# Mean square spread by a constant matrix, inverse root on VectorE, in a three-stage fp32 kernel

## The reference, cut to what matters

```
qn, kn = q / norm over rows, k / norm over rows
a = softmax(kn.T @ qn / tau)                 # 256 x 256
x = v @ a                                    # 6016 x 256
x = x / sqrt(mean(x*x over the 256) + 1e-6) * rms_g
g = x @ w1_gate;  y = (g * sigmoid(g) * (x @ w1_val)) @ w1_out
out = (sigmoid(y @ w2_gate) * (y @ w2_val)) @ w2_out
```

## Time and profile before

| what | value |
|---|---|
| device time, median of 3 runs | 1309.73 us (1309.46 to 1310.09) |
| span of the profiled execution | 1307.8 us |
| PE busy | 1295.0 us, 99% |
| DVE busy | 655.3 us, 50% |
| ACT busy | 455.3 us, 35% |
| POOL busy | 37.7 us, 3% |

### The profile page before, as it was taken

One profiled execution on the slowest core, in us unless ns is written; L12 is line 12 of the kernel. 1 busy time (PEld: TensorE's weight loads), 2 busy tenths in 40 slices (PEclk: granted clock), 3 DMA queues, 4 the chain that ended last, 5 costly groups with the idle time before them and its releaser, 6 DMA issues.

```text
span 1307.8 us, 15519 instructions
## 1 busy us (share of the span) xinstructions
PE 1295.0 (99%) x5706; PEld 1067.3 (82%) x5706; DVE 655.3 (50%) x1014; ACT 455.3 (35%) x737; POOL 37.7 (3%) x32
## 2 busy tenths in 40 slices
PE   8999999999999999999999999999999999999998
PEld 7878888888888888888888888888888888889888
DVE  6776544544554554554454455455455455445333
ACT  5453533333332333333333333333333333333322
POOL 0000500000000000000000000000000000000000
PEclk9999999999999999999999999999999999999999
DMA  9910000100100100010010010010010001000000
GB/s 345 315 57 1 1 1 1 33 0 0 32 0 0 32 0 0 8 24 0 0 32 0 0 32 0 0 32 0 0 25 7 0 0 28 1 1 17 1 17 13
DMA packets 60569, 34.43 MB, mean 26 GB/s; under 512 B 50816, under 2 KB 54144, under 8 KB 60544
## 3 DMA queue, kind: packets, MB, share of 16 engines
q1 hardware_dynamic: 60544, 34.09, 8.9%
HBM read 27.92 MB, written 6.16 MB: 26 GB/s over the span
## 4 chain that ended last, share of the span: by engine, by line
PE 98%; DVE 1%; DMA 0%; SPq 0%; POOL 0%; issue 0%; ACT 0%; DVEq 0%
PE ps L661 21%; PE ps L662 21%; PE ps L663 21%; PE ps L779 10%; PE ps L780 10%; PE ps L781 10%; PE ps L727 3%; PE ps L687 1%; DMA qk<-in_k 0%; PE ps L696 0%; PE ps L703 0%; SPq L250 0%; POOL small L296 0%; PE ps L713 0%; DVE w_lo_v L442 0%
## 5 line engine op out<-in xcount | busy, mean ns | idle before, releaser
L596 DVE TENSOR_TENSOR h<-ps,h 128x512 f32<-128x512 f32 (+1 forms) x288 | 196.1, 681 | 328.0 <-PE ps L663 322.2
L390 ACT ACTIVATE h_hi<-h 128x512 fp32r<-128x512 f32 (+1 forms) x288 | 179.6, 624 | 406.9 <-DVE h L596 405.3
L384 ACT ACTIVATE h<-ps 128x512 f32<-128x512 f32 (+1 forms) x288 | 169.9, 590 | 402.5 <-PE ps L663 402.5
L601 DVE TENSOR_TENSOR h_lo<-h,h_hi 128x512 fp32r<-128x512 f32 (+1 forms) x288 | 195.4, 679 | 131.0 <-ACT h_hi L390 127.1
L779 PE MATMUL ps<-h_hi,w_hi_o 128*128 128x512 f32 (+1 forms) x576 | 225.9, 392 | 0.0
L780 PE MATMUL ps<-h_lo,w_hi_o 128*128 128x512 f32 (+1 forms) x576 | 225.8, 392 | 0.0
L781 PE MATMUL ps<-h_hi,w_lo_o 128*128 128x512 f32 (+1 forms) x576 | 225.3, 391 | 0.0
L592 DVE TENSOR_TENSOR h<-ps,h 128x512 f32<-128x512 f32 (+1 forms) x144 | 98.0, 681 | 165.5 <-ACT h L384 164.8
L781 PEld LDWEIGHTS ps<-h_hi,w_lo_o 128*128 128x128 f32 x576 | 110.8, 192 | 23.0
L779 PEld LDWEIGHTS ps<-h_hi,w_hi_o 128*128 128x128 f32 x576 | 110.2, 191 | 23.6
L780 PEld LDWEIGHTS ps<-h_lo,w_hi_o 128*128 128x128 f32 x576 | 110.1, 191 | 21.9
(11 more groups left out here) (111 smaller groups left out, 1321.6 us busy)
## 6 DMA issues: line engine op xcount, KB each, us to landing
v_in<-in_v SPq DMA_DIRECT2D x44, 128.0 KB, 3.2
out<-out_sb SPq DMA_DIRECT2D x44, 128.0 KB, 2.6
qk<-in_q SPq DMA_DIRECT2D x10, 512.0 KB, 7.6
qk<-in_k SPq DMA_DIRECT2D x10, 512.0 KB, 9.1
w_raw_g<-in_moe_w_gate SPq DMA_DIRECT2D x6, 512.0 KB, 7.9
w_raw_v<-in_moe_w_val SPq DMA_DIRECT2D x6, 512.0 KB, 8.0
w_raw_o<-in_moe_w_out SPq DMA_DIRECT2D x6, 512.0 KB, 9.0
qk<-in_q SPq DMA_DIRECT2D x3, 256.0 KB, 2.9
```

Of the source, the lines that this page charges most:

```text
L384: nc.scalar.activation(h[:, slot, 0:w], ps[:, GATE[slot], 0:w], ACT.Sigmoid).then_inc(sig_done, 1)
L390: nc.scalar.activation(h_hi[:, part, 0:w], h[:, slot, 0:w], ACT.Copy).then_inc(hi_done, 1)
L596: nc.vector.tensor_tensor(h[:, slot, 0:w], ps[:, VALUE[slot], 0:w], h[:, slot, 0:w], ALU.mult).then_inc(h_done, 1)
L601: nc.vector.tensor_tensor(h_lo[:, part, 0:w], h[:, slot, 0:w], h_hi[:, part, 0:w].bitcast(F32), ALU.subtract).then_inc(lo_done, 1)
```

## The change

From block 2 on, `add_squares` is followed by a split of the summed squares (`squares_high` on ACT, `squares_low` on DVE). Two matmuls of w columns with a 128x128 matrix of 1/256 as weights (`spread_mean`) put the mean square of each token on all partitions. ACT copies it to SBUF with 1e-6 added (`mean_copy`). DVE makes a first guess of the inverse root from the bits (`root_seed`, on integers), and betters it in three rounds of three instructions (`root_better`). `x_norm` then reads it from SBUF. `sum_squares`, `mean_square`, the power on POOL, `diagonal` and `spread_rms` are left for blocks 0 and 1 alone. The steps in which the pieces stand are moved too, for block 1 as well: `vt_high` and `vt_low` from 1 to 0, `make_x` from 2 to 1, `x_square`, `x_gain` and `add_squares` from 3 to 2, `sum_squares` from 4 to 3, `mean_square`, `diagonal` and `spread_rms` from 5, 6, 7 to 4, 5, 6, `x_norm` from 8 to 9, both `xs_low` to 10. `spread_mean` stands in step 4, `mean_copy` and `root_seed` in 5, the three rounds in 6, 7 and 8. Two tiles are added in SBUF, `mean_r` and `root`.

```diff
@@ -59,6 +61,10 @@
+    def narrow(b):
+        return isinstance(b, int) and b < 2
     def width(b):
@@ -117,12 +123,14 @@
+        mean_r = sb("mean_r", [P, P], F32R)
...
+        root = sb("root", [P, 2, BLOCK])
@@ -302,9 +312,6 @@
                                         ALU.subtract).then_inc(w_lo2_done, 1)
-            with pool.Fori(0, FULL - 2) as b:
-                inverse_rms(b + 2)
-            inverse_rms(FULL)
@@ -336,6 +343,18 @@
                 nc.scalar.activation(sq[:, c, 0:w], ps[:, X[c], 0:w], ACT.Square).then_inc(x_squared, 1)
+            def squares_high(b, dst):
+                w = width(b)
+                act.wait_ge(squares_added, b)
+                nc.scalar.activation(dst[0][:, 0, 0:w], sq[:, 0, 0:w], ACT.Copy).then_inc(sq_hi_done, 1)
+            def mean_copy(b):
+                w = width(b)
+                act.wait_ge(ms_spread, b - 1)
+                nc.scalar.activation(sq[:, 0, 0:w], ps[:, X[0], 0:w], ACT.Copy, bias=1e-6).then_inc(ms_copied, 1)
@@ -392,8 +411,11 @@
             def next_x(mid, end, b, vt):
-                mid[1] = [(vt_high, b, c, vt) for c in range(CC)]
-                mid[3] = [(x_square, b, c) for c in range(CC)]
+                mid[0] = [(vt_high, b, c, vt) for c in range(CC)]
+                mid[2] = [(x_square, b, c) for c in range(CC)]
+                if not narrow(b):
+                    mid[3] = [(squares_high, b, vt)]
+                    mid[5] = [(mean_copy, b)]
@@ -511,12 +533,44 @@
+            def squares_low(b, dst):
+                w = width(b)
+                dve.wait_ge(sq_hi_done, b - 1)
+                nc.vector.tensor_tensor(dst[1][:, 0, 0:w], sq[:, 0, 0:w], dst[0][:, 0, 0:w].bitcast(F32), ALU.subtract)\
+                  .then_inc(sq_lo_done, 1)
+            def root_seed(b):
+                w = width(b)
+                dve.wait_ge(ms_copied, b - 1)
+                nc.vector.tensor_scalar(root[:, 0, 0:w].bitcast(I32), sq[:, 0, 0:w].bitcast(I32), -0.5, float(0x5f3759df),
+                                        ALU.mult, ALU.add).then_inc(root_step, 1)
+            def root_better(b, n):
+                w = width(b)
+                steps = (b - 2) * (1 + 3 * ROOT_ROUNDS) + 1 + 3 * n
+                y, t = root[:, 0, 0:w], root[:, 1, 0:w]
+                dve.wait_ge(root_step, steps)
+                nc.vector.scalar_tensor_tensor(out=t, in0=y, scalar=-0.5, in1=y, op0=ALU.mult, op1=ALU.mult)\
+                  .then_inc(root_step, 1)
+                dve.wait_ge(root_step, steps + 1)
+                nc.vector.tensor_tensor(t, t, sq[:, 0, 0:w], ALU.mult).then_inc(root_step, 1)
+                dve.wait_ge(root_step, steps + 2)
+                nc.vector.scalar_tensor_tensor(out=y, in0=t, scalar=1.5, in1=y, op0=ALU.add, op1=ALU.mult)\
+                  .then_inc(root_step, 1)
             def x_norm(b, c):
                 w = width(b)
-                dve.wait_ge(rinv_spread, b + 1)
+                if narrow(b):
+                    dve.wait_ge(rinv_spread, b + 1)
+                    by = ps[:, X[1], 0:w]
+                else:
+                    dve.wait_ge(root_step, (b - 1) * (1 + 3 * ROOT_ROUNDS))
+                    by = root[:, 0, 0:w]
                 dve.wait_ge(xg_done, b * 2 + c + 1)
-                nc.vector.tensor_tensor(x_raw[:, c, 0:w], x_raw[:, c, 0:w], ps[:, X[1], 0:w], ALU.mult)\
-                  .then_inc(xn_done, 1)
+                nc.vector.tensor_tensor(x_raw[:, c, 0:w], x_raw[:, c, 0:w], by, ALU.mult).then_inc(xn_done, 1)
@@ -572,6 +626,7 @@
             nc.vector.tensor_copy(ones_r[:, :], ones[:, :]).then_inc(ones_r_done, 1)
+            nc.vector.tensor_scalar(mean_r[:, :], ones[:, :], 1.0 / C, None, ALU.mult).then_inc(mean_r_done, 1)
             dve.wait_ge(g_loaded, 16)
@@ -604,14 +659,16 @@
             def next_x(extras, b, vt):
-                for j, work in {0: [(turn_v, b, 0), (turn_v, b, 1)],
-                                1: [(vt_low, b, 0, vt), (vt_low, b, 1, vt)],
-                                3: [(x_gain, b, 0), (x_gain, b, 1), (add_squares, b)],
-                                5: [(mean_square, b)],
-                                6: [(diagonal, b, vt)],
-                                8: [(x_norm, b, 0), (x_norm, b, 1)]}.items():
-                    extras[j] = extras.get(j, []) + work
+                work = {0: [(turn_v, b, 0), (turn_v, b, 1), (vt_low, b, 0, vt), (vt_low, b, 1, vt)],
+                        2: [(x_gain, b, 0), (x_gain, b, 1), (add_squares, b)]}
+                if narrow(b):
+                    work |= {4: [(mean_square, b)], 5: [(diagonal, b, vt)]}
+                else:
+                    work |= {3: [(squares_low, b, vt)], 5: [(root_seed, b)]}
+                    work |= {6 + n: [(root_better, b, n)] for n in range(ROOT_ROUNDS)}
+                work[9] = [(x_norm, b, 0), (x_norm, b, 1)]
+                for j in work:
+                    extras[j] = extras.get(j, []) + work[j]
             class Walk:
@@ -637,8 +694,7 @@
                         next_x(extras, b + 2, xs)
-                        extras[9] = [(xs_low, b + 2, 0)]
-                        extras[10] = [(xs_low, b + 2, 1)]
+                        extras[10] = [(xs_low, b + 2, c) for c in range(CC)]
                     layer(seq2(b), width(b), None, extras,
@@ -687,6 +743,17 @@
                 mm.then_inc(ms_made, 1)
+            def spread_mean(b, squares):
+                w = width(b)
+                pe.wait_ge(mean_r_done, 1)
+                pe.wait_ge(xg_done, b * 2 + 1)
+                pe.wait_ge(sq_hi_done, b - 1)
+                nc.tensor.matmul(ps[:, X[0], 0:w], mean_r[:, :], squares[0][:, 0, 0:w], start=True, stop=False)
+                pe.wait_ge(sq_lo_done, b - 1)
+                nc.tensor.matmul(ps[:, X[0], 0:w], mean_r[:, :], squares[1][:, 0, 0:w], start=False, stop=True)\
+                  .then_inc(ms_spread, 1)
@@ -834,11 +901,13 @@
                 def next_x(self, j, b, vt):
-                    if j == 2:
+                    if j == 1:
                         make_x(b, vt)
-                    if j == 4:
+                    if j == 3 and narrow(b):
                         sum_squares(b)
-                    if j == 7:
+                    if j == 4 and not narrow(b):
+                        spread_mean(b, vt)
+                    if j == 6 and narrow(b):
                         spread_rms(b, vt)
```

More of the change, by code:

```diff
@@ L25 @@
 F32R = mybir.dt.float32r
+I32 = mybir.dt.int32
 ALU = mybir.AluOpType
@@ L36 @@
 GROUPS = 3
+ROOT_ROUNDS = 3
 def build(nc, q, k, v, tau, rms_g, w1_gate, w1_val, w1_out, w2_gate, w2_val, w2_out, out):
@@ L181, in build @@
         diag_done, rinv_spread, xn_done = sem("diag_done"), sem("rinv_spread"), sem("xn_done")
+        mean_r_done, sq_hi_done, sq_lo_done = sem("mean_r_done"), sem("sq_hi_done"), sem("sq_lo_done")
+        ms_spread, ms_copied, root_step = sem("ms_spread"), sem("ms_copied"), sem("root_step")
         xs_hi_done, xs_lo_done = sem("xs_hi_done"), sem("xs_lo_done")
```

## The result

The changed kernel takes 1302.21 us (median of four runs, 1301.89 to 1304.48) where the kernel before takes 1309.91: a ratio of 0.9945, 95% interval 0.9931 to 0.996. The prediction was 1301.9. A later direct repeat gave 1302.02 us and 0.9942 (0.9929 to 0.9955). The span went from 1307.8 to 1300.2 us, with 1300.0 predicted.

The account below looks back on a forecast made before the run. PE, busy 99% and waiting for nobody in the loop, was taken as the bound: 8.7 us won on the sums less 0.9 at the start, 7.8 off 1309.73, gives 1301.9 us, range 1300.3 to 1304.3.

Parts of the forecast that it names:

- Part 1: Small column-sum matmuls leave PE's stream: 0.89 us for each of blocks 2 to 10, 0.67 for the tail, 8.7 together.
- The upper end of 10.8: Bound on the gain from the removed sums, counting the whole 1.12 us, ordinary matmul included, for each block.
- Part 2: `spread_mean` in step 4 costs PE the same 0.47 us as `spread_rms` in step 7: balance zero, at least 3 us left.
- Part 3: DVE's added work per block, nine round instructions at 0.72 us, 6.5 us in steps 6 to 8, stays hidden from PE.
- the deadline that was worked out: In the loop, the down needs DVE's low part 8.4 us after its value; DVE may be 4.7 us late.
- Part 4: ACT's two added copies of 128x512, about 0.62 us each, in steps 3 and 5 cost zero, even with table loads.
- Part 5: Moved steps in the loop cost zero; `make_x` behind step 1 has 2.0 us left.
- Part 6: Layer 1 of block 0: waits for `vt_low` and `low_weight` lose 0.9 us, bounds 0 to 2.5.
- The pace of PE: Rival, 13%: new places in SBUF and busier engines shift the downs' pace in the loop, giving 1303.5 or 1298.7 us.
- The start was not free: Judges the rival, 8%, that DVE's queue in block 0 catches up and the start costs nothing: 1301.0 us.
- `make_x` too early: Rival, 4%: in step 1 of prepared passes PE waits for turned, split v; at 3.5 us of chain 15 us lost, 1317.
- Nothing removed: Rival, 2%: the sums in PE's stream were hidden before, so no gain: 1309.7 to 1310.6 us.

Follow-up runs that it names:

- places alone: The kernel before with the two new tiles allocated and never used, so later tiles in SBUF lie where the change puts them: 1309.96 us, ratio 1.0005.

## Why the prediction was right

**The whole:** 7.8 us forecast, 7.7 by the medians; from the first up of layer 1 to the last matmul it is 1225.7 us (68.25 to 1293.98) instead of 1233.5 (68.16 to 1301.68), again 7.8. The path was right, PE's own stream and the two waits in block 0. That the sum came out to the tenth is in part luck: the turns won a little less than forecast and the start lost a little less.

**Part 1, the sums:** 8.7 us forecast, 8.6 found: nine turns of 0.88 and 0.67 for the tail. Doubling them showed that they stand exposed, and widening them that the price is the pair's and not the columns'. One size inside it was off: a pair is 0.11 us, not 0.10 with a slow start behind. The 107 ns of the Trainium skill ("TensorE: Matmul & The Clock Gate", "LDWEIGHTS (loading the stationary operand)") are 4 ns under the 111 measured, so that rule was nearer than my reading of the row, while the sum of 8.7 was nearer than the 8.3 by the rule. The upper end of 10.8 should have been 11.0, as it takes the tail without its ordinary matmul; nothing hangs on it.

**Part 2, the spread:** 0.47 for 0.47, no wait on it. DVE's split of the squares ends at 400.89 and the spread starts at 404.89, so 4.0 us were left, of at least 3 forecast.

**Part 3, DVE.** A pass of the rounds, with its seed (DVE in time):

```profile
409.06 0.42 DVE L547 TENSOR_SCALAR root<-scratch 128x512 int32<-128x512 int32 x1
...
412.65 0.69 DVE L651 TENSOR_TENSOR h<-ps,h 128x512 f32<-128x512 f32 x1 [2.12 <-PE ps L719]
413.26 0.68 DVE L556 SCALAR_TENSOR_TENSOR root<-root 128x512 f32<-128x512 f32 x1
413.97 0.69 DVE L559 TENSOR_TENSOR root<-root,scratch 128x512 f32<-128x512 f32 x1
414.70 0.69 DVE L561 SCALAR_TENSOR_TENSOR root<-root 128x512 f32<-128x512 f32 x1
415.31 0.68 DVE L656 TENSOR_TENSOR h_lo<-h,h_hi 128x512 fp32r<-128x512 f32 x1
```

Chained instructions start 0.71 to 0.73 apart, as taken from the earlier trace rows; those that don't need each other 0.61 (412.65 and 413.26, 414.70 and 415.31). The kind with a scalar is no slower than a plain one at this size (0.69); I had given it 0.78. The seed is 0.42. In all DVE is busy 53 us more, not 60: 72 us for the rounds, the seeds and the splits, less 18 for what was removed. The Trainium skill ("VectorE: DVE Perf Modes", "The DRAIN you can't avoid"), read as adding a flush to each, gave 1.1 us apart; the traces have 0.72, also over twelve in a row, so here it is not to be added to the duration. That DVE's time is free was tested from both sides and holds, up to the deadline that was worked out.

**Part 4, ACT.** The copy with a constant takes 0.59 us, and the profile has two loads of a table as before; zero, as said.

**Part 5, the moves in the loop:** zero forecast; turns of 105.29 against 105.27 with the moves alone, 0.2 us in all. The margin of `make_x` came out as counted: subtractions from 386.25 and the first matmul at 389.60 in the changed kernel, so 2.1 us.

```profile
386.25 1.29 DVE L486 TENSOR_TENSOR xs_lo<-x_raw,xs_hi 128x512 fp32r<-128x512 f32 x2
```

```profile
389.60 0.40 PE L717 MATMUL ps<-xs_hi,a_hi 128*128 128x512 f32 x1
```

**Part 6, the start:** 0.9 forecast and 0.81 found. Each station came within 0.1 us: `make_x` at 74.69 (74.6), step 4 at 87.47 (87.4), step 5 at 91.79 (91.7). What was off is the station at which the loss was read: before, step 5 began with the end of the last small pair still to come, 0.08 us, which the moved sums no longer put there. Undoing the moves for block 1 alone gave the same 0.81 back.

**The rivals.** The pace of PE in the loop did not move (places alone: 105.26); that of the tail's layer 1 differs by 0.6 us between executions of one kernel, so it is not the change's. The start was not free. `make_x` too early needed a later split to come true, and then cost 0.81 a pass and a slow first matmul. "Nothing removed" is refuted by the doubled sums. Left open: why the downs of steps 2 to 5 of a prepared pass are shorter (1.38 us against 1.42). They are so in both kernels, and no run here tells why.

## What to carry to other kernels

Where one engine is busy 99% of the time and waits for nobody, count what it issues by start times: here a pair of a weight load and a matmul of one column cost 0.11 us, half of a matmul of 512 columns. It paid to take eight such pairs off PE in each block, at the price of some 5 us more of work on DVE, which was idle half of the time. Price the other engines by deadline, not by busy share: two tiles of lag gave DVE 8.4 us to deliver, and it used 8.0 without loss, while with three more instructions PE waited 1.6 us in every pass. And look at the first pass by itself: moves that cost 0.03 us a turn in the loop cost 0.8 us once where that lag was not yet built up.

## What the runs showed of the hardware that I had not expected

A pair of an fp32 weight load of 128x128 and a small matmul takes 0.11 us on PE whether the matmul has 1 column or 64. At 128x512 fp32 on DVE, SCALAR_TENSOR_TENSOR costs what TENSOR_TENSOR does (0.69 us), and a TENSOR_SCALAR on int32 from SBUF 0.42. Instructions of 128x512 start 0.72 us apart where each needs the last one, and 0.61 where it doesn't. In two of the profiled executions the granted clock was 0.50 for a stretch around 10.5 to 13.8 us, and PE had waited 1.9 to 2.3 us for q and k just before; the 160 matmuls that began there took 36.4 to 36.5 us instead of 34.8. Layer 1 of the tail took either 38.2 or 38.7 us, in executions of one and the same kernel.
